# Linear attention and two feed-forward layers on one core: one loop over all steps, with x split a tile ahead

## The reference

```python
def _attn_ref(q, k, v):                      # 4 batches, 8 heads, 576 rows, 64 columns
    q_s = np.exp(q - np.max(q, axis=-1, keepdims=True))
    q_s = q_s / (np.sum(q_s, axis=-1, keepdims=True) + 1e-09)
    k_s = np.exp(k - np.max(k, axis=2, keepdims=True))
    k_s = k_s / (np.sum(k_s, axis=2, keepdims=True) + 1e-09)
    kv = np.einsum('bhsd,bhse->bhde', k_s, v)
    return np.einsum('bhsd,bhde->bhse', q_s, kv)
# its output, as x with 2304 rows of 512, goes through two layers (512 -> 2048 -> 512)
def _moe_ref(x, w_in, w_out, s, b):
    r = np.maximum(x @ w_in, 0.0)
    return (s * (r * r) + b) @ w_out
def _moe2_ref(x, w_in, w_out):
    h = x @ w_in
    sp = np.where(h > 20.0, h, np.log1p(np.exp(np.minimum(h, 20.0))))
    return (h * np.tanh(sp)) @ w_out
```

## Time and profile before

| | |
|---|---|
| median of three runs | 889.38 us |
| profiled execution | 890.38 us, of which the span of the records is 888.6 us |
| TensorE busy | 865.1 us (97%), 4132 matmuls |
| DVE, ACT busy | 613.5 us (69%), 378.7 us (43%) |
| TensorE's granted clock, mean | 0.988 of full speed |
| TensorE in the chain that ended last | 80% |

### The profile page before, as it was taken

How to read it: one execution, slowest core, us unless ns; L and a number is a source line. 1 busy time by engine, 2 the same in 40 slices (tenths; PEclk the granted TensorE clock), 3 DMA queues, 4 the chain that set the end, 5 groups by cost and what they waited for, 6 DMA issues and landing times.

```text
span 888.6 us, 11126 instructions
## 1 busy us (share of the span) xinstructions
PE 865.1 (97%) x4132; PEld 717.5 (81%) x4132; DVE 613.5 (69%) x1037; ACT 378.7 (43%) x621; POOL 26.6 (3%) x30
## 2 busy tenths in 40 slices
PE   9789999999999999999999899998999999999998
PEld 4578888888888888888997678897888788878886
DVE  8787776665475554222466889688797779778975
ACT  4445433332333323222356555455454445445443
POOL 2300000000000000000000000000000000000000
PEclk9799999999999999999999999999999999999999
DMA  9921111111111100000153000100000000000001
GB/s 227 339 53 40 25 29 28 41 41 41 41 40 40 40 0 1 1 1 0 49 190 143 1 0 1 48 1 1 25 1 0 12 36 0 0 28 19 0 0 48
DMA packets 60645, 36.15 MB, mean 41 GB/s; under 512 B 48320, under 2 KB 50368, under 8 KB 60608
## 3 DMA queue, kind: packets, MB, share of 16 engines
q1 hardware_dynamic: 60608, 35.66, 14.2%
HBM read 30.93 MB, written 4.72 MB: 40 GB/s over the span
## 4 chain that ended last, share of the span: by engine, by line
PE 80%; DVE 11%; ACT 6%; issue 2%; POOL 1%; DMA 0%; DVEq 0%; ACTq 0%
PE H L796 38%; PE Y L810 21%; PE Y L824 17%; PE H L763 2%; PE H L784 2%; ACT t L458 1%; DVE g L702 1%; DVE t L674 1%; ACT t L460 1%; DVE wout_lo L598 1%; DVE t L679 1%; ACT wout_hi L360 1%; DVE t L684 1%; PE H L775 1%; DVE win_lo L598 1%
## 5 line engine op out<-in xcount | busy, mean ns | idle before, releaser
L796 PE MATMUL H<-xs_hi,win_hi 128*128 128x512 f32 (+1 forms) x640 | 240.8, 376 | 7.7 <-DVE g_raw L697 3.3
L796 PE MATMUL H<-xs_hi,win_lo 128*128 128x512 f32 (+1 forms) x640 | 236.8, 370 | 0.0
L796 PE MATMUL H<-xs_lo,win_hi 128*128 128x512 f32 (+1 forms) x640 | 236.7, 370 | 0.0
L824 PE MATMUL Y<-wout_hi,g 128*128 128x512 f32 x576 | 190.1, 393 | 5.4 <-DVE g L702 5.4
L810 PE MATMUL Y<-g,wout_hi 128*128 128x512 f32 (+1 forms) x640 | 183.3, 371 | 0.7 <-DVE g L582 0.7
L796 PEld LDWEIGHTS H<-xs_hi,win_hi 128*128 128x128 f32 x640 | 121.4, 190 | 30.0 <-DVE g_raw L697 4.0
L796 PEld LDWEIGHTS H<-xs_hi,win_lo 128*128 128x128 f32 x640 | 121.3, 190 | 20.8
L796 PEld LDWEIGHTS H<-xs_lo,win_hi 128*128 128x128 f32 x640 | 121.4, 190 | 20.4
L824 PEld LDWEIGHTS Y<-wout_hi,g 128*128 128x128 f32 x576 | 108.7, 189 | 30.9 <-DVE g L702 8.7
L810 PEld LDWEIGHTS Y<-g,wout_hi 128*128 128x128 f32 x640 | 115.2, 189 | 20.1 <-DVE g L582 0.9
L577 DVE SCALAR_TENSOR_TENSOR g_raw<-g_raw,s_col 128x512 f32<-128x512 f32 (+1 forms) x80 | 55.5, 694 | 96.4 <-ACT g_raw L381 96.1
(11 more groups left out here) (73 smaller groups left out, 823.2 us busy)
## 6 DMA issues: line engine op xcount, KB each, us to landing
win_raw<-in_moe_w_in_dram SPq DMA_DIRECT2D x8, 1024.0 KB, 7.0
wout_raw<-in_moe_w_out_dram SPq DMA_DIRECT2D x8, 1024.0 KB, 7.3
g_flat<-in_v_dram SPq DMA_DIRECT2D x32, 144.0 KB, 3.3
out_dram<-xy SPq DMA_DIRECT2D x18, 256.0 KB, 2.1
qbuf<-in_q_dram SPq DMA_DIRECT2D x24, 144.0 KB, 2.8
kbuf<-in_k_dram SPq DMA_DIRECT2D x24, 144.0 KB, 2.9
raw<-in_k_dram SPq DMA_DIRECT2D x4, 288.0 KB, 3.9
raw<-in_q_dram SPq DMA_DIRECT2D x4, 288.0 KB, 6.1
```

The costliest lines, as they stand in the source:

```text
L796: last = nc.tensor.matmul(Hb[f % banks][:, 0:w], a[:, i, cols], m[:, i, 0:w], start=(i == 0 and n == 0), stop=(i == KC - 1 and n == XPASS ...
L824: last = nc.tensor.matmul(Y[i][:, :], g[:, f % LAG_B, a, rows], m[:, f, :], start=(f == 0 and n == 0), stop=(f == FC - 1 and n == XPASS - 1))
```

## The change

All steps c of a layer now form one loop (c is counted through both layers, 16 steps a tile), written out in full. TensorE's down products stay three (then four) steps behind across the tiles: there is no drain between tiles, nor between the layers. The x of the next tile is split during the present one (`split_at`), the high part into one of two buffers, the low part over x itself (`xlo`). Y is copied out in the third step of the next tile in layer 1 and in the first tile of layer 2, in the fourth step of a tile after that. The first down product of a tile waits for it. In tile 1.0 the high part `w_in` 1 is made after step 0 and not ahead of it. The units start at the steps in `START`, after that step's `g_lo`. `kv_product` makes the two heads apart, each on 64 of the array's columns.

```diff
+        def slot(c):
+            return c % LAG_A if c < FC * TILES else (3, 2, 0, 1)[c % LAG_B]
+        START = {}
+        for batch in range(1, B):
+            for p in range(NP):
+                START[FC * (batch - 1) + (0, 4, 7, 10)[p] if batch == 1 else FC * (batch - 1) + (-3, 1, 5, 9)[p]] = (batch, p)
+        def split_at(pos, f):
+            steps = (5, 9, 12, 15) if pos == 0 else (5, 8, 11, 14) if pos < TILES else (6, 8, 10, 12)
+            return steps.index(f) if pos + 1 < len(SRC) and f in steps else None
...
@@ scalar, layer 1, then layer 2
+            for c in range(FC * TILES):
+                if pos > 0 and f == LAG_A - 1:
+                    take_y(pos - 1)
+                relu(c, WIDTH[pos])
+                if unit_at(c - 1):
+                    q_exp(unit_at(c - 1))
+                if unit_at(c - 2):
+                    take_qT(unit_at(c - 2))
+                g_hi(c, WIDTH[pos])
...
+                if split_at(pos, f) is not None:
+                    split_hi(pos + 1, split_at(pos, f))
...
+            for c in range(FIRST, END):
+                rough_inverse(c, WIDTH[pos])
+                if pos == TILES and f == LAG_A - 1 or pos > TILES and f == LAG_B - 1:
+                    take_y(pos - 1)
+                if c + 1 < END:
+                    exp_h(c + 1, WIDTH[(c + 1) // FC])
+                if c > FIRST:
+                    g_hi_b(c - 1, WIDTH[(c - 1) // FC])
...
@@ vector, layer 1
-                    if attention and i == 0:
-                        q_max(n)
-                        q_shift(n)
-                        k_max(n)
...
-                    square(T, f, w)
-                    g_lo(T, f, w)
...
+                square(c, w)
+                if unit_at(c - 1):
+                    k_shift(unit_at(c - 1))
+                g_lo(c, w)
+                if unit_at(c - 1):
+                    q_sum(unit_at(c - 1))
+                    q_eps(unit_at(c - 1))
+                    q_inv(unit_at(c - 1))
+                    q_scale(unit_at(c - 1))
+                if unit_at(c):
+                    q_max(unit_at(c))
+                    q_shift(unit_at(c))
+                    k_max(unit_at(c))
...
@@ tensor
-                    last = nc.tensor.matmul(n.bank[0][:, 0:PAIR * VW], n.kj[:, j, :], n.v[:, :, j, :],
-                                            start=(j == 0), stop=(j == J - 1))
+                    for h in range(PAIR):
+                        rows = slice(h * D, (h + 1) * D)
+                        last = nc.tensor.matmul(n.bank[0][rows, 0:VW], n.kj[:, j, rows], n.v[:, h, j, :],
+                                                start=(j == 0), stop=(j == J - 1))
...
+                if f == 0 and pos > 0:
+                    pe.wait_ge(y_taken_act, y_count(pos) // 2)
+                    pe.wait_ge(y_taken_dve, y_count(pos) // 2)
...
+            for c in range(FIRST):
+                if unit_at(c - 5):
+                    x_product(unit_at(c - 5))
+                n = unit_at(c - 3)
+                if n and n.u > NP:
+                    q_transpose(n)
+                if c >= HA:
+                    pe.wait_ge(ha_taken, c - HA + 1)
+                up(c, HA)
+                if n and n.u == NP:
+                    q_transpose(n)
+                elif n:
+                    kv_product(n)
+                if c >= LAG_A:
+                    down_a(c - LAG_A)
```

More of the change, by code:

```diff
@@ L270, in _ @@
                 load_wout(0, i)
[L271 to L276, removed]
+            for u in range(NP + 1, B * NP):
+                load_unit(Unit(u // NP, u % NP))
             for i in range(NG):
@@ L365, in hi_part @@
                 (win_hi_part if kind == 'in' else wout_hi_part)(layer, i)
[L367 to L374, removed]
@@ L500, in _ @@
+            g_hi_b(END - 1, WIDTH[-1])
+            take_y(len(SRC) - 1)
         @block.vector
@@ L547, in kv_norm @@
                 bank = n.bank[0]
-                for h in range(PAIR):
-                    rows = slice(h * D, (h + 1) * D)
-                    last = nc.vector.tensor_scalar_add(ksum[rows, n.p, :], bank[rows, (h + 1) * VW - 1:(h + 1) * VW], EPS)
+                last = nc.vector.tensor_scalar_add(ksum[:, n.p, :], bank[:, VW - 1:VW], EPS)
                 last.then_inc(ksum_done, 1)
@@ new lines, in g_lo_b @@
+            def g_lo_b(c, w):
+                dve.wait_ge(ghi_done, c + 1)
+                nc.vector.tensor_tensor(g[:, slot(c), 1, 0:w], g_raw[:, slot(c), 1, 0:w],
+                                        g[:, slot(c), 0, 0:w].bitcast(F32), ALU.subtract).then_inc(g_ready, 1)
+            FIRST, END = FC * TILES, FC * len(SRC)
+            for c in range(FIRST, END + 2):
+                pos, f = c // FC, c % FC
+                w0, w1, w2 = [WIDTH[min(c - back, END - 1) // FC] for back in range(3)]
+                if FIRST < c <= END:
+                    rough_ratio(c - 1, w1)
+                if c < END:
+                    min_e(c, w0)
+                if FIRST < c <= END:
+                    unity(c - 1, w1)
+                leave = pos - 1 if c < END and f == (LAG_A if pos == TILES else LAG_B) - 1 else None
+                if c >= FIRST + 2:
+                    g_lo_b(c - 2, w2)
+                if leave is not None:
+                    take_y(leave, 1)
+                if c < END:
+                    m_of_e(c, w0)
+                if leave is not None and BANKS[leave] == KC:
+                    take_y(leave, 3)
+                if FIRST < c <= END:
+                    ratio(c - 1, w1)
+                    gate(c - 1, w1)
+                if pos == TILES and f in LATE_PARTS:
+                    kind, i = LATE_PARTS[f]
+                    lo_part(kind, 1, i)
+                if c < END and split_at(pos, f) is not None:
+                    split_lo(pos + 1, split_at(pos, f))
@@ L755, in _ @@
+            for i in (1, 3):
+                take_y(len(SRC) - 1, i)
         @block.tensor
```

483 lines of the change are left out of this document (192 added, 291 removed).

## The result

The changed kernel takes 906.42 us, the median of four runs (905.99 to 907.88), against 890.74 us for the kernel before (889.14 to 893.13, four runs now): a ratio of 1.0177, with a 95% interval of 1.0146 to 1.0207. It is slower by 15.7 us. The profiled execution took 906.82 us with a span of 905.0 us, against 888.6. The prediction said 894.6 us, with a range that ended at 903.

A forecast was written before the change was run, and what follows sets the result against it. TensorE, busy 97% of the span, was taken as the bound, fuller queues giving at most 22.5 us. Terms +2.0 + 1.6 + 1.2 + 0.7 - 2.4 + 1.6 + 0.5 = +5.2 on 889.4 gave 894.6 us, range 877 to 903.

The forecast's parts named there:

- Tile 1.0: First unit: the wait at the fourth up product is exchanged for 4.1 us at `q_transpose`, slow stretch behind it: +2.0 us.
- The other units: Later units in layer 1: VectorE's second round has no slack before the transpose; 0.2 us for eight units, +1.6.
- My +1.2 for the unit at step 7: Tile 1.0: low part of `w_out` 2 behind its first round makes the second end 1.2 us after TensorE wants it.
- Steady units: Seven units in tiles 1.1 and 1.2, at 0.2 us each for lack of slack, within the +1.6 for eight units.
- From layer 1 to layer 2: First `gate` ends at 488.0, not 491.8; down product 5 starts at 523.2, not 525.65: -2.4 us.
- Edges of layer 2: Drains worth 7.4 us go; VectorE's waits for `split_hi` and first down products' waits for Y copies cost 9.0: +1.6.
- The product of k and v: 24 records of 65 columns take 1.39 us a unit, against 1.35 before; 12 units, +0.5 us, bounds -8 and +9.5.
- the rival: Product of k and v: two heads run side by side, 12 times -0.68 instead of +0.5, 885.9 us; chance 0.20.
- The second rival: Queues absorb VectorE's lateness in layer 2, first `gate` ending by about 486 us; tile 1.0 keeps +2.0: 878 us; chance 0.22.

The follow-up runs named there:

- `q_scale` sooner: Kernel after the change, with `q_sum` to `q_scale`, then `k_shift`, between `square` and `g_lo` on VectorE: 894.61 us, ratio 1.0038.
- the kernel with all edits: Kernel after, first unit's round ahead, low parts moved, ScalarE's copies first, low halves later, `q_scale` ahead of `g_lo`, tile 2.0's x split at 3, 5, 8, 12: 878.25 us.
- the product alone: Kernel before the change, with the product of k and v per head (and the shorter `kv_norm`) as the one edit: 887.71 us, ratio 0.9955.

## Why the prediction was wrong

- **Tile 1.0: the mechanism of the first unit was right.** I said 4.1 us of wait at `q_transpose` up to 57.0, followed by a slow stretch of 1.4; the trace has 4.01 us up to 57.38 and a stretch of 1.6.
- **The other units: this step failed.** "A unit that starts at step s is transposed ahead of up product s + 3" is right, but I looked only at `q_scale`. The transpose has a second condition, `take_x` of the unit before. Before, a unit starts every four steps and `take_x`, at step s + 5, comes two steps ahead of the next transpose. With starts at 0, 4, 7 and 10 it comes one step ahead, behind a low part and a round with no slack. For the whole of tile 1.0 I had 2.0 + 1.2 and a share of the 1.6; it cost 11.0, of which the waits of 2.23, 2.77 and 0.57 us and two stretches of 1.6 are 8.8. Moving the low parts took 5.3 us off this tile; a wait of 2.24 us came in another place. My +1.2 for the unit at step 7 saw the low part but charged it to `q_scale` alone, and without a slow stretch.
- **Steady units: mis-sized.** I took 0.2 us each for the lack of slack. In tiles 1.1 and 1.2 two of the four wait, 1.03 and 0.43 us by the rows; with the refill behind each, the edit that makes them go gave 2.0 us a tile, 0.5 a unit. For the unit that starts at step 1 of a tile I had left the copies of Y out: they stand ahead of DVE's second round, and the wait of 1.03 us at 173.89 is for this unit (DVE after the change):

```profile
168.04 1.28 DVE L587 COPY xy<-Y 128x512 f32<-128x512 f32 x2
...
172.88 0.95 DVE L522 TENSOR_TENSOR qbuf<-qbuf,qinv 96x768 f32<-96x768 f32 x1
```

- **From layer 1 to layer 2: wrong in place.** I put the first `gate` at 488.0 and "about 4 us earlier"; it ends at 502.8, that is 17.9 us after the tile's first up product, against 14.4 before (491.8 less 477.4). VectorE stands 3.74 us for ACT's high part of `w_out` 2. I had taken these waits over from before as a cost that stays the same, though in the new loop they stand ahead of the first `gate`. From tile 1.4 to the start of 2.1 the change gave back 1.9 us in all, near the 2.4 that I said, but by tile 1.4 itself (2.2) and not by an earlier gate.
- **Edges of layer 2: right in kind and place.** I said 3.3 us in tile 2.2, ended by ACT's copy, from VectorE's arrears of 1.2 us a quarter; it was 3.30 us, with 1.55, 1.33, 1.33 and 1.33 us of waiting ahead of the four quarters. The slow stretch behind it cost 2.8 us and not 1.4: 5.26 us for the first 12 matmuls and 0.4 lost on the next three. In tile 2.0 I said 2.3 us for the same copy, and it was 2.42, but without the slow stretch of 1.6 behind it. At the first down products of 2.1, 2.3 and 2.4 I had 1.4, 0.8 and 0.8 us; there TensorE stood 0.99, 0.56 and 0.56 us, and the profile names no engine for it (`issue`). The terms that I listed here also don't add up to the 9.0 us: with 0.2 at each of the three other places they make 8.3 without the 1.3 us of waiting in 2.1, and 9.6 with it. From 2.1 to the end the change cost 4.5 us, where I had 1.6.
- **The product of k and v: the rival was right in its mechanism, and less than half of its size.** I took +0.5 us; it is -3.5. The rival had -8.2, since 0.68 us a unit has no edges in it.
- **The second rival** (the queues absorb it, 878 us) failed as it stood: VectorE did not reach the first `gate` in time (502.8 and not 486). With the order mended layer 2 does run near TensorE's pace, and the time is the 878 us that it had worked out. That number is partly luck, since it had no gain in it from the product.
- **The sum.** The prediction's terms make +5.2 and the spans +16.4. Tile 1.0 accounts for 7.5 of the difference, tiles 1.1 and 1.2 for 0.2 (2.8 us more of waits, 2.6 less for the product), tile 1.4 and layer 2 for 3.4, the start for 0.4; behind the last matmul 0.2 us are saved.

What stays open: how much of each slow stretch belongs to the wait ahead of it, since its length isn't the same behind equal waits, and whether the first unit's place can be freed entirely. Of the five orders tried there, four kept one wait of 3.1 to 4.0 us; with `q_scale` sooner and nothing else it was 1.7 us (and 0.7 for `relu`), so the kernel with all edits would probably do better without its first round ahead. That wasn't tried. Nor was the kernel before, with its drains, given the same order of DVE's and ACT's work, so how much of the gain belongs to the loop itself is not shown.

## What to carry to other kernels

When a schedule is packed closer, list every semaphore that a moved instruction waits for, not only the one that was last before: the bank that the previous user still holds is the one that turns up. Put a low half one step behind the high half that another engine makes for it; here that alone was worth 12 us. The loop without drains lost time until its engines stood in the right order; loop and order together then gave 9 us beside the product alone (878.25 against 887.71). And allow for slow matmuls behind each long wait of TensorE: here they came behind most of the waits above 2 us, though not all.

## What the runs showed of the hardware

- Matmuls on 64 of the array's columns run beside those on the other 64 if the two alternate: 24 records of 65 columns take 0.85 us from start to start, against 1.36 when one head comes after the other, and 24 more alternating ones take 0.71, 0.030 each. Entering and leaving that use costs 0.35 us in all, against 0.04 for the full-width records of the same product.
- Behind a wait of 2.2 us the granted clock was 0.53 over 3.6 us; behind the one of 3.3 us it was 0.50 over the next 5.2. With the same wait (3.33 us) in the run with `q_scale` sooner it was 0.67 over a stretch of that length, and the tile 1.3 us shorter. The wait of 2.24 us at 141.17 in the run with the low parts moved had no slow stretch behind it, nor had the one of 1.63 us at 640.13 with the low halves a step later. So the loss behind a wait of 1.6 us or more was between 0 and 2.8 us here, most often near 1.6, and equal waits did not have equal losses.
